# Attention without its division: the row sums' reciprocals kept in memory and applied to x where the feed-forward layer reads it

## The chip, the cores and the metric

The kernel runs on one core of one Trainium2 chip. The metric is the device time of one execution in microseconds (us), as the median of several runs. The core has a matrix engine (TensorE, PE), a vector engine (VectorE, DVE), a scalar engine (ScalarE, ACT), a general engine (GpSimd, POOL) and SyncE (SP), which here only issues DMA transfers. Each engine works through its own list of instructions in order; semaphores join the lists.

## The reference

```python
# attention: q, k, v are (4, 8, 576, 64); masked in blocks of 64
scores = scale * np.matmul(q, k.transpose(0, 1, 3, 2))
scores = np.where(mask, scores, -1000000000.0)
attn = np.exp(scores - np.max(scores, axis=-1, keepdims=True))
attn = attn / (np.sum(attn, axis=-1, keepdims=True) + 1e-09)
attn_out = np.matmul(attn, v)
x = attn_out.transpose(0, 2, 1, 3).reshape(2304, 512)
# feed-forward: w_in (512, 2048), w_out (2048, 512)
h = x @ w_in
g = np.where(h > 0.0, h, np.exp(np.minimum(h, 0.0)) - 1.0)
x = g @ w_out
# experts: one of 8 for each token where x @ w_skip > 0
out = x; out[do] = x[do] + gate * (relu(x[do] @ w1[e]) @ w2[e])
```

All of it is in float32.

## The kernel before

**Attention.** Two heads of a batch are a pair; there are 16 pairs, 4 for each of the 4 batches. One step of each engine's loop works on pair n and finishes the two pairs before it: TensorE makes the scores of n, turns the exponentials of n-1 and multiplies those of n-2 with v (`values`). ScalarE makes the exponentials with their row sums. VectorE makes the row maxima, the reciprocals of the row sums (`recips`), and copies turned tiles. The exponentials aren't divided. Instead the reciprocals, 9 columns of 128, are turned by TensorE and copied to `r_rows` (9 x 128, `recip_rows`), SyncE stores them to memory (`store_recips`, line 263) and loads them back repeated over the 64 partitions of each head into `r_sb` (`load_recips`, lines 271 and 274, four loads), and VectorE's `final` (line 443) multiplies the pair's sums in `o_ps` with `r_sb` into `attn_sb`, which SyncE stores to `attn_t` (line 257). `attn_t` is x turned: 512 rows (columns of x), 2304 tokens. There is one `o_ps`, one `r_sb` and one `attn_sb`, and TensorE may write the next `o_ps` only after `final` (`out_done`).

SyncE's step (`step` in `sync`) issues in this order: the part of w_in for this pair (line 279), q and k of pair n+3 (line 231, four loads), v of pair n (lines 250 and 252, three), the store of the reciprocals of n-1, the store of `attn_sb` of n-2, the four loads of reciprocals of n-1. GpSimd's step splits q and k of pair n+1 in a high and a low part (`qk_hi`, `qk_lo`, lines 343 and 346) and then the part of w_in (`wi_hi`, `wi_lo`, lines 354 and 359). TensorE's scores of a pair wait for its split.

**Feed-forward.** It runs over 6 blocks of 384 tokens. x of a block is loaded from `attn_t` in four row groups (`x_raw`, `load_x_rows`, line 35) and split in `xt_hi` (ScalarE, line 1537) and `xt_lo` (GpSimd, line 1137); for block 0 GpSimd does both within the attention's last steps (`x_parts`, lines 372 and 375). A block has 16 chunks f of the hidden layer. TensorE makes the hidden product of chunk f (`ff_hidden`, `h_ps`) and then the output product of chunk f-2 (`ff_output`, `out_ps`). ScalarE makes the exponential (`ex`, line 1520) and VectorE the rest and the low half `gt` (lines 1359, 1362, 1352). In block 0 w_out is loaded chunk by chunk (`load_wo`, line 1052, four buffers `w_raw`) and split by ScalarE (`wo_hi`, line 1585, two chunks ahead, ahead of that step's exponential in its list) and GpSimd (`wo_lo`). x of block b+1 is split at chunks 4, 6, 8 and 10 of block b (`X_AT`). The experts follow.

```python
        def final(n, i):
            wait(dve, pv_done, n + 1)
            wait(dve, r_in, R_LOADS * (n + 1))
            wait(dve, stored[1 - i], 16 * ((n + i) // 2))
            dve.tensor_tensor(attn_sb[:, :], o_ps[:, O0:O0 + S], r_sb[:, :], ALU.mult)\
               .then_inc(out_done, 1)
```

Of the kernel before, what the change touches and what calls it, by code (L numbers as in the profile page):

```python
# [21 lines left out]
P = 128  # L22
# [43 lines left out]

def attention_engines(nc, ctx, place, attn_t, wi, x_raw, x_in, xt0, x_hi_done, x_lo_done):

# [28 lines left out]
    WO, XT1, GT = LATER_AT  # L97
    R_LOADS = 64
    PIECES = [(j, max(j * P, a), b) for j in range(T) for a, b in ((0, O_SPLIT), (O_SPLIT, S)) if j * P < b]
# [4 lines left out]
    def sb(name, shape, dt):  # L104
        return place.enter_context(nc.sbuf_tensor(name, shape, dt))
# [33 lines left out]
    prob4 = sb("prob4", [P, S], F32)  # L139
    r_sb = sb("r_sb", [P, S], F32)  # L140
    vb.append(sb("v1", [P, T, 2, D], F32))
# [6 lines left out]
    half_row = sb("half_row", [P, P], BF16)  # L148

    r_dram = [nc.dram_tensor(f"recip_rows{i}", (COLS, P), F32, kind="Internal").ap() for i in range(2)]  # L150

# [23 lines left out]
    r_stored = sem("r_stored")  # L175
    r_in = sem("r_in")
    pv_done = sem("pv_done")
# [62 lines left out]
    def sync(sp, first_wo, next_wo):  # L240
# [19 lines left out]
        def store_recips(n, i):  # L260

            wait(sp, r_row_done, n + 1)
            sp.dma_start(r_dram[i], r_rows[:, :]).then_inc(r_stored, 16)

        def load_recips(n, i):

            wait(sp, out_done, n)
            wait(sp, r_stored, 16 * n + 16)
            for h in range(2):
                rows = HALVES[h]  # L270
                sp.dma_start(r_sb[rows, 0:FULL * P], r_dram[i][h * FULL:(h + 1) * FULL, :]  # L271
                             .rearrange("(o u) q -> o (u q)", o=1).broadcast_to([D, FULL * P]))\
                  .then_inc(r_in, 16)
                sp.dma_start(r_sb[rows, FULL * P:S], r_dram[i][COLS - 1:COLS, rows]  # L274
                             .broadcast_to([D, TAIL])).then_inc(r_in, 16)

# [5 lines left out]
        def step(kk, i):  # L282
            now, past, older, ahead = pair(kk, i), pair(kk, i, -1), pair(kk, i, -2), pair(kk, i, 3)
            first = isinstance(kk, int) and kk <= 0
            if now and not (first and now[0] == 0):
                load_wi(now[0])
            if ahead:
                load_qk(*ahead)
            if now and not first:
                load_v(*now)  # L290
            if past:
                store_recips(*past)
            if older:
# [25 lines left out]
        store(PAIRS - 2, 0)  # L319
        load_recips(PAIRS - 1, 1)  # L320
        next_wo()
        store(PAIRS - 1, 1)

    def gpsimd(pool):
# [60 lines left out]
    def vector(dve):  # L385
# [96 lines left out]

        all_pairs(step, -1, PAIRS + 1)(dve)
        return lambda: final(PAIRS - 1, 1)
# [84 lines left out]
    def tensor(pe, hidden):  # L569
# [138 lines left out]
        for m in range(PAIRS - 2, PAIRS):  # L708
# [12 lines left out]
    return dict(sync=sync, gpsimd=gpsimd, vector=vector, scalar=scalar, tensor=tensor, stored=stored,  # L721
                out_done=out_done, pv_done=pv_done, pairs=PAIRS, turned=tails_turned)

# [8 lines left out]
def experts(nc, x2_rows, table, meta, w1, w2, out, w1_raw, w1_in):  # L732
# [42 lines left out]
    with ExitStack() as ctx:  # L775
# [12 lines left out]

        x_hi_done, x_lo_done = sem("x_hi_done"), sem("x_lo_done")
        with ExitStack() as place:  # L790
# [5 lines left out]
            attend = attention_engines(nc, ctx, place, attn_t, wi, x_raw, xr_in, xt0, x_hi_done, x_lo_done)  # L796
# [4 lines left out]
        wo_raw = [spare[:, r // 2, r % 2] for r in range(WR)]  # L801
        ex = sb("ex", [P, 2, NB], F32)
        x2 = [sb(f"x2_{s}", [P, DM], F32) for s in range(TB)]
# [206 lines left out]
        def _(sp):  # L1010
            def load_x(b, ks=range(KC)):

                for k in ks:
                    wait(sp, x_lo_done, KC * (b - 1) + k + 1)
                    load_x_rows(sp, attn_t, k, b * NB, x_raw, xr_in)

            def store_x2(b):
# [46 lines left out]
            for stored in attend["stored"]:  # L1064
                sp.wait_ge(stored, 16 * attend["pairs"] // 2)
            load_x(1)
            load_gates()
            for f in range(2 * WR, FC):
# [157 lines left out]
        def _(dve):  # L1226
# [128 lines left out]
            def step(b, f):  # L1355
# [159 lines left out]
        def _(act):  # L1515
# [14 lines left out]
            def x_hi(b, k):  # L1530
                act.wait_ge(xr_in[k], 16 * (b + 1))
                if k == 0:
# [422 lines left out]
```

## Time and profile before

| | |
|---|---|
| median of 3 runs | 811.36 us (811.15 to 812.75) |
| the profiled execution | 812.12 us, span 810.3 us |
| busy, share of the span: PE, DVE, ACT, POOL | 94%, 63%, 43%, 30% |
| attention (to the last `r_rows` copy) | to 182.8 us |
| feed-forward, then experts | to about 617 us, then to the end |
| mean granted TensorE clock | 0.983 of full speed |
| DMA queue of SyncE (q1) | 96928 packets, 81.89 MB |

The profiled execution is 0.8 us above the median of the runs. The span is the time from the first to the last instruction of it. Times in the rows below are us from the start of the span. [...] A matmul counts as busy for longer when the clock is low, so a busy share doesn't tell a slow clock from work.

### The profile page before, as it was taken

The page shows a single profiled execution, that of the slowest core. Times are in us where ns is not written, and L with a number is a line of the kernel's source. Part 1 is how long each engine was busy: PE and PEld are TensorE (multiplying, and loading weights), DVE is VectorE, ACT ScalarE, POOL GpSimd, SP SyncE. Part 2 cuts the span into 40 slices and gives each one's busy share as a digit, 9 for nine tenths or more (in the row PEclk, how much of TensorE's full clock was granted, in tenths as well). Part 3 has the DMA queues.
Part 4 walks back from the last instruction along what each step waited for, and adds up shares of the span by engine and source line. Part 5 has one row for each costly group of instructions (what it writes and reads, how often), then busy time and mean ns, then how long its engine had stood idle before and what let it go on. Part 6 is the DMA issues. An engine that isn't in the chain of part 4 may idle for free.

```text
span 810.3 us, 15508 instructions
## 1 busy us (share of the span) xinstructions
PE 765.6 (94%) x5170; PEld 645.9 (80%) x5171; DVE 511.3 (63%) x1307; ACT 349.9 (43%) x830; POOL 245.3 (30%) x240
## 2 busy tenths in 40 slices
PE   5998888889999999999999999999997999999995
PEld 3777766668889888888988888898875777878884
DVE  3877677564333885687488488526755898377242
ACT  4877776663433222321322322223442776256241
POOL 4876676764440120120121012000112223213111
PEclk9999999799999999999999999999998999999999
DMA  9566666555252020210210200321333699164000
GB/s 159 141 166 168 161 166 181 134 154 150 77 179 79 20 72 1 89 30 1 78 30 11 79 1 27 121 88 53 112 131 105 225 334 352 46 225 149 26 21 9
DMA packets 102405, 88.16 MB, mean 109 GB/s; under 512 B 66164, under 2 KB 77828, under 8 KB 102224
## 3 DMA queue, kind: packets, MB, share of 16 engines
q1 hardware_dynamic: 96928, 81.89, 33.4%
q0 software_dynamic: 3056, 5.00, 1.8%
q10 hardware_dynamic: 2368, 0.59, 0.4%
q8 instruction: 30, 0.49, 0.2%
q14 instruction: 23, 0.19, 0.1%
HBM read 72.26 MB, written 18.34 MB: 112 GB/s over the span
## 4 chain that ended last, share of the span: by engine, by line
PE 77%; SPq 9%; DMA 4%; issue 4%; DVE 3%; ACT 1%; POOL 1%; DVEq 1%; POOLq 0%; ACTq 0%
PE h_ps L1695 12%; PE out_ps L1695 12%; PE h_ps L1696 11%; PE h_ps L1697 11%; PE out_ps L1697 11%; PE out_ps L1696 11%; SPq L231 3%; DMA recip_rows<-r_rows 3%; PE o_ps L672 2%; SPq L274 2%; SPq L271 1%; PE out_ps L1831 1%; SPq L250 1%; SPq L252 1%; PE o_ps L581 1%
## 5 line engine op out<-in xcount | busy, mean ns | idle before, releaser
L1520 ACT ACTIVATE ex<-h_ps 128x384 f32<-128x384 f32 x96 | 47.3, 493 | 272.4 <-PE h_ps L1697 272.4
L1695 PE MATMUL h_ps<-xt_hi,wi_hi 128*128 128x384 f32 x384 | 131.9, 343 | 0.2 <-POOL xt_lo L375 0.2
L1696 PE MATMUL h_ps<-xt_lo,wi_hi 128*128 128x384 f32 x384 | 129.7, 338 | 0.0
L1697 PE MATMUL h_ps<-xt_hi,wi_lo 128*128 128x384 f32 x384 | 129.7, 338 | 0.0
L1359 DVE TENSOR_SCALAR ex<-ex 128x384 f32<-128x384 f32 x96 | 37.0, 385 | 138.7 <-ACT ex L1520 137.5
L1695 PE MATMUL out_ps<-wo_hi,gt 128*128 128x512 f32 x288 | 114.5, 398 | 0.0
L1697 PE MATMUL out_ps<-wo_hi,gt 128*128 128x512 f32 x288 | 113.9, 395 | 0.0
L1696 PE MATMUL out_ps<-wo_lo,gt 128*128 128x512 f32 x288 | 113.3, 393 | 0.0
L529 ACT ACTIVATE prob<-s_ps,negmax 128x128 f32<-128x128 f32 (+2 forms) x144 | 77.8, 554 | 25.6 <-DVE negmax L391 23.9
L1241 DVE CUSTOM_DVE_ANT_0 x2t<-x,w_raw 128x512 bf16<-128x512 f32 x108 | 82.7, 806 | 0.4
L1137 POOL TENSOR_TENSOR xt_lo<-x_raw,xt_hi 128x384 fp32r<-128x384 f32 x20 | 28.3, 1416 | 156.2 <-ACT xt_hi L1537 156.1
L1695 PEld LDWEIGHTS h_ps<-xt_hi,wi_hi 128*128 128x128 f32 x384 | 72.2, 188 | 4.0 <-POOL xt_lo L375 0.5
L1696 PEld LDWEIGHTS h_ps<-xt_lo,wi_hi 128*128 128x128 f32 x384 | 72.2, 188 | 3.1
L1145 POOL DMA_INDIRECT route_table<-entry,slot x18 | 20.9, 1164 | 177.2 <-DVE slot L1320 161.0
L1697 PEld LDWEIGHTS h_ps<-xt_hi,wi_lo 128*128 128x128 f32 x384 | 72.1, 188 | 0.0
L1697 PEld LDWEIGHTS out_ps<-wo_hi,gt 128*128 128x128 f32 x288 | 54.1, 188 | 13.4
L1695 PEld LDWEIGHTS out_ps<-wo_hi,gt 128*128 128x128 f32 x288 | 54.1, 188 | 9.1 <-DVE gt L1352 0.8
L1696 PEld LDWEIGHTS out_ps<-wo_lo,gt 128*128 128x128 f32 x288 | 54.1, 188 | 8.9
L391 DVE TENSOR_REDUCE negmax<-s_ps 128x2 f32<-128x256 f32 (+1 forms) x64 | 50.8, 816 | 15.3 <-PE s_ps L659 15.2
L1362 DVE TENSOR_TENSOR ex<-h_ps,ex 128x384 f32<-128x384 f32 x96 | 53.5, 558 | 3.3
L1695 PE MATMUL out_ps<-wo_hi,ht_hi 128*128 128x512 f32 x120 | 50.3, 419 | 3.7 <-DVE ht_lo L1428 3.5
L1352 DVE TENSOR_TENSOR gt<-ex,gt 128x384 fp32r<-128x384 f32 x96 | 53.1, 554 | 0.0
(179 smaller groups left out, 1587.6 us busy)
## 6 DMA issues: line engine op xcount, KB each, us to landing
w_raw<-in_moe_w_dram SPq DMA_DIRECT2D x56, 512.0 KB, 4.8
raw_qk<-in_q_dram SPq DMA_DIRECT2D x32, 144.0 KB, 3.2
attn_t<-attn_sb SPq DMA_DIRECT2D x16, 288.0 KB, 2.2
x_raw<-attn_t SPq DMA_DIRECT2D x24, 192.0 KB, 2.4
out_dram<-x SPq DMA_DIRECT2D x18, 256.0 KB, 2.1
x_rows<-x SPq DMA_DIRECT2D x18, 256.0 KB, 2.4
v<-in_v_dram SPq DMA_DIRECT2D x32, 128.0 KB, 2.9
wi_raw<-in_moe_w_in_dram SPq DMA_DIRECT2D x16, 256.0 KB, 2.9
```

The costliest lines, as they stand in the source:

```text
L231: eng.dma_start(raw[i][rows, :, h, :], heads_of(t, n)[h].rearrange("(b p) d -> p b d", p=D))\
L391: dve.tensor_reduce(heads_cols(negmax, u), s_pair(u), AX_X, ALU.max, negate=True).then_inc(max_done, 1)
L529: act.activation(dst, src, ACT.Exp, bias=negmax[:, c:c + 1], accum_out=rowsum[i][:, c:c + 1]).then_inc(exp_done, 1)
L1137: pool.tensor_tensor(xtk(b % 2, 1, k), x_raw[k][:, :], xtk(b % 2, 0, k).bitcast(F32), ALU.subtract).then_inc(x_lo_done, 1)
L1241: ins = dve.tensor_tensor_reduce(dot_rows[:, ((E + 1) * t + e) % 2], x2[s][:, :], all_skip if e == E else all_gates[:, e, :], 1.0, 0.0, AL ...
L1352: dve.tensor_tensor(gt[:, f % 2, 1], ex[:, f % 2], gt[:, f % 2, 0].bitcast(F32), ALU.subtract).then_inc(g_lo_done, 1)
L1359: dve.tensor_scalar(e, e, 1.0, -1.0, ALU.min, ALU.add).then_inc(em_done, 1)
L1362: dve.tensor_tensor(e, h_ps[:, f % 2, 0:NB], e, ALU.max).then_inc(g_done, 1)
L1520: act.activation(ex[:, f % 2], h_ps[:, f % 2, 0:NB], ACT.Exp).then_inc(ex_done, 1)
L1695: pe.matmul(dst, stat[0], mov[0], start=start, stop=False, skip_group_check=True)
L1696: pe.matmul(dst, stat[0], mov[1], start=False, stop=False, skip_group_check=True)
L1697: return pe.matmul(dst, stat[1], mov[0], start=False, stop=stop, skip_group_check=True)
```

## The change

`final` becomes a copy: `attn_t` now holds undivided sums. The reciprocals of all pairs are kept in one array in memory, `recip_rows`, with a row of 9 x 128 for each pair. `load_recips` of the attention is gone with its four loads for each pair. Where x of a block has been loaded, SyncE loads the reciprocals of its tokens and of the two heads of that row group, repeated over 64 partitions for each head (`recip_row`, a new `load_recips`), and VectorE multiplies `x_raw` with them in place (`normalise`, 128 x 384, 24 times in all). ScalarE and GpSimd split x only after that (`x_norm`). A block's tokens lie in one, two or three pieces of `recip_rows`: block 0 and 3 need one load for each row group, block 2 and 5 two, block 1 and 4 three. Blocks 0 and 1 have a buffer for each row group (in `w1_raw`), the others one buffer for all four.

```diff
+def recip_row(r_rows, b, k):
+    PAIR_TOKENS, MAIN = 576, 512
+    for batch in range(4):
+        first = batch * PAIR_TOKENS
+        for a, z, at in ((0, MAIN, 0), (MAIN, PAIR_TOKENS, 2 * MAIN)):
+            lo, hi = max(first + a, b * X_TILES * P), min(first + z, (b + 1) * X_TILES * P)
+            if lo < hi:
+                row = r_rows[4 * batch + k:4 * batch + k + 1, at:at + 2 * (z - a)]
+                yield (slice(lo - b * X_TILES * P, hi - b * X_TILES * P),
+                       row.rearrange("o (h q) -> h o q", h=2)[:, :, lo - first - a:hi - first - a]
+                       .broadcast_to([2, P // 2, hi - lo]))
+def load_recips(sp, r_rows, b, k, dst, x_r_in):
+    for cols, src in recip_row(r_rows, b, k):
+        sp.dma_start(dst[:, cols], src).then_inc(x_r_in[min(b, 2)][k], 16)
+def normalise(dve, x, r, x_in, x_r_in, x_norm, b, k, loads):
+    dve.wait_ge(x_in[k], 16 * (b + 1))
+    dve.wait_ge(x_r_in[min(b, 2)][k], 16 * loads)
+    dve.tensor_tensor(x[k][:, :], x[k][:, :], r, ALU.mult).then_inc(x_norm, 1)
...
-            sp.dma_start(r_dram[i], r_rows[:, :]).then_inc(r_stored, 16)
-        def load_recips(n, i):
-            wait(sp, out_done, n)
-            wait(sp, r_stored, 16 * n + 16)
-            for h in range(2):
...
+            sp.dma_start(r_all[bass.ds(n, 1)].rearrange("o (c q) -> (o c) q", q=P), r_rows[:, :])\
+              .then_inc(r_stored, 16)
...
-            wait(dve, r_in, R_LOADS * (n + 1))
-            dve.tensor_tensor(attn_sb[:, :], o_ps[:, O0:O0 + S], r_sb[:, :], ALU.mult)\
-               .then_inc(out_done, 1)
+            dve.tensor_copy(attn_sb[:, :], o_ps[:, O0:O0 + S]).then_inc(out_done, 1)
...
-                pool.wait_ge(x_in[k], 16)
+                pool.wait_ge(x_norm, k + 1)
...
+            for k in range(KC):
+                load_r(1, k)
             load_gates()
...
+                for k in range(KC):
+                    if b and b < LAST and k < KC - 1:
+                        load_r(b + 1, k + 1)
+                    if b + 2 < BLOCKS:
+                        load_x(b + 2, [k])
                 if b + 2 < BLOCKS:
-                    load_x(b + 2)
+                    load_r(b + 2, 0)
...
+                if b < LAST and f + 1 in X_AT:
+                    k = X_AT.index(f + 1)
+                    normalise(dve, x_raw, x_r[b + 1][k], xr_in, x_r_in, x_norm, b + 1, k,
+                              recip_loads(r_all, b + 1, k))
...
-                act.wait_ge(xr_in[k], 16 * (b + 1))
+                act.wait_ge(x_norm, KC * b + k + 1)
```

SyncE's list at the head of pair 12 of the attention, before: the four loads of x of block 0, then the pair's own transfers. "128x384" is what one transfer writes, x3 that three follow each other, and "waits" names the semaphores.

```order
L35 DMA x_raw<-attn_t 128x384 [waits stored1,stored0]
L35 DMA x_raw<-attn_t 128x384 x3
L279 DMA wi_raw<-in_moe_w_in_dram 128x4x128 [waits wi_lo_done]
L231 DMA raw_qk<-in_q_dram 64x9x64 [waits tails_turned]
L231 DMA raw_qk<-in_q_dram 64x9x64
L231 DMA raw_qk<-in_k_dram 64x9x64 x2
L250 DMA v<-in_v_dram 128x4x64 [waits pv_done]
L250 DMA v<-in_v_dram 128x4x64
L252 DMA v<-in_v_dram 64x2x64
L263 DMA recip_rows<-r_rows 9x128 [waits r_row_done]
L257 DMA attn_t<-attn_sb 128x576 [waits out_done]
L271 DMA r_sb<-recip_rows 64x512 [waits r_stored,out_done]
```

The same place now. "w_raw<-recip_rows" are the new loads (the names of the buffers have lost their numbers, here it is `w1_raw`).

```order
L35 DMA x_raw<-attn_t 128x384 [waits stored1,stored0]
L35 DMA x_raw<-attn_t 128x384 x3
L85 DMA w_raw<-recip_rows 128x1x384 [waits r_stored]
L85 DMA w_raw<-recip_rows 128x1x384 x3
L300 DMA wi_raw<-in_moe_w_in_dram 128x4x128 [waits wi_lo_done]
L263 DMA raw_qk<-in_q_dram 64x9x64 [waits tails_turned]
L263 DMA raw_qk<-in_q_dram 64x9x64
L263 DMA raw_qk<-in_k_dram 64x9x64 x2
L282 DMA v<-in_v_dram 128x4x64 [waits pv_done]
L282 DMA v<-in_v_dram 128x4x64
L284 DMA v<-in_v_dram 64x2x64
L295 DMA recip_rows<-r_rows 9x128 [waits r_row_done]
```

Four new loads stand between the loads of x and the pair's own, and none follows the pair's stores.

SyncE's list after the attention now, from the last store of `attn_sb` to the loads of w_out's chunks from 8 on. Before, the loads of `gates` came right behind those of x.

```order
L289 DMA attn_t<-attn_sb 128x576 [waits out_done]
L35 DMA x_raw<-attn_t 128x384 [waits r_stored,x_lo_done,stored1,stored0]
L35 DMA x_raw<-attn_t 128x384 [waits x_lo_done] x3
L85 DMA w_raw<-recip_rows 128x1x128
L85 DMA w_raw<-recip_rows 128x1x64
L85 DMA w_raw<-recip_rows 128x1x192
...
L1075 DMA gates<-in_moe_w_gate_dram 128x4x8
L1076 DMA gates<-in_moe_w_skip_dram 128x4x1
L1092 DMA w_raw<-in_moe_w_out_dram 128x512 [waits wo_lo_done] x8
```

The three loads of the middle come four times, once for each row group: twelve transfers have been put ahead of w_out's.

## Rows read from the trace of the kernel before

**Rows 1.** The page's chain that ended last, by engine.

```profile
PE 77%; SPq 9%; DMA 4%; issue 4%; DVE 3%; ACT 1%; POOL 1%; DVEq 1%; POOLq 0%; ACTq 0%
```

**Rows 2.** Timeline of SyncE's queue, one pair: start, us, line, transfer.

```profile
94.21 0.39 SPq L279 DMA_DIRECT2D wi_raw<-in_moe_w_in_dram  x1
...
100.16 0.40 SPq L263 DMA_DIRECT2D recip_rows<-r_rows  x1
...
101.86 0.51 SPq L271 DMA_DIRECT2D r_sb<-recip_rows  x1
...
104.56 0.39 SPq L279 DMA_DIRECT2D wi_raw<-in_moe_w_in_dram  x1
```

**Rows 3.** Waits of the whole span: us in total, times, longest.

```profile
DVE attn_sb L443 <- DMA r_sb<-recip_rows: 18.0, 10, 3.1
```

**Rows 4.** Busy time by stretches: length, PE, PEld, DVE, ACT, POOL, PEclk, DMA.

```profile
23.95:51.07 27.12, 26.42 (x406) 20.48 (x404) 22.25 (x48) 23.52 (x78) 23.76 (x20) 1.00 0.63 151
...
94.71:104.45 9.74, 9.03 (x138) 7.00 (x135) 7.60 (x17) 7.70 (x26) 7.21 (x7) 1.00 0.64 165
...
136.44:148.25 11.81, 10.33 (x138) 8.44 (x136) 7.76 (x16) 7.80 (x27) 6.75 (x6) 0.86 0.94 196
148.25:162.29 14.04, 11.03 (x136) 8.89 (x134) 7.88 (x17) 7.76 (x26) 9.34 (x8) 0.76 0.41 121
```

**Rows 5.** Timeline of VectorE: copies of `r_rows`, one `final` between them.

```profile
51.07 0.28 DVE L427 COPY r_rows<-t_ps 9x128 f32<-9x128 f32 x1 [1.01 <-PE t_ps L581]
...
63.70 0.76 DVE L443 TENSOR_TENSOR attn_sb<-o_ps,r_sb 128x576 f32<-128x576 f32 x1 [2.04 <-DMA r_sb<-recip_rows]
...
136.44 0.28 DVE L427 COPY r_rows<-t_ps 9x128 f32<-9x128 f32 x1 [1.00 <-PE t_ps L581]
```

**Rows 6.** DMA in three stretches: 269 to 272, 182.9 to 185.2, 228.6 to 231.

```profile
DMA packets 144, 0.20 MB, mean 66 GB/s; under 512 B 16, under 2 KB 144, under 8 KB 144
...
q1 hardware_dynamic: 144, 0.20, 23.2%
...
x_raw<-attn_t SPq DMA_DIRECT2D x1, 192.0 KB, 2.2
...
DMA packets 72, 0.13 MB, mean 59 GB/s; under 512 B 9, under 2 KB 18, under 8 KB 71
...
DMA packets 160, 0.28 MB, mean 116 GB/s; under 512 B 24, under 2 KB 24, under 8 KB 160
```

**Rows 7.** The table by stretches again, a large load: last columns DMA share, GB/s.

```profile
232.40:238.00 5.60, 5.60 (x29) 4.96 (x28) 1.99 (x5) 2.33 (x5) 1.67 (x2) 1.00 0.91 342
```

**Rows 8.** Timeline of GpSimd: w_in's part, then the split of the next pair.

```profile
142.59 1.04 POOL L354 TENSOR_TENSOR wi_hi<-wi_raw,one 128x512 f32 x1 [4.73 <-DMA wi_raw<-in_moe_w_in_dram]
...
145.11 1.04 POOL L343 TENSOR_TENSOR qk_hi<-qk_f,one 128x512 fp32r<-128x512 f32 x1
...
148.90 1.67 POOL L346 TENSOR_TENSOR qk_lo<-qk_f,qk_hi 128x704 fp32r<-128x704 f32 x1
```

**Rows 9.** Timeline of VectorE in block 1 of the feed-forward.

```profile
283.69 0.36 DVE L1359 TENSOR_SCALAR ex<-ex 128x384 f32<-128x384 f32 x1 [0.27 <-ACT ex L1520]
...
284.56 0.55 DVE L1352 TENSOR_TENSOR gt<-ex,gt 128x384 fp32r<-128x384 f32 x1
```

**Rows 10.** Timelines at the attention's end: VectorE, GpSimd, TensorE.

```profile
174.56 1.00 DVE L435 COPY pt<-t_ps 128x384 f32<-128x384 f32 x2
...
174.54 0.83 POOL L372 TENSOR_TENSOR xt_hi<-x_raw,one 128x384 fp32r<-128x384 f32 x1
...
178.37 0.44 PE L1695 MATMUL h_ps<-xt_hi,wi_hi 128*128 128x384 f32 x1 [0.22 <-POOL xt_lo L375]
```

**Rows 11.** Timelines behind the attention: TensorE's last values, ScalarE's list.

```profile
184.96 2.93 PE L672 MATMUL o_ps<-pt,v 128*64 128x256 f32 x28
...
203.61 0.62 ACT L1585 ACTIVATE wo_hi<-w_raw 128x512 fp32r<-128x512 f32 x1
...
207.00 0.49 ACT L1520 ACTIVATE ex<-h_ps 128x384 f32<-128x384 f32 x1 [2.76 <-PE h_ps L1697]
```

More of the change, by code:

```diff
@@ L64, in attention, with recip_loads, attention_engines @@
     given.update(q=q, k=k, v=v, w_in=w_in)
-def attention_engines(nc, ctx, place, attn_t, wi, x_raw, x_in, xt0, x_hi_done, x_lo_done):
+def recip_row(r_rows, b, k):
[12 more added lines that the diff above has]
+        sp.dma_start(dst[:, cols], src).then_inc(x_r_in[min(b, 2)][k], 16)
+def recip_loads(r_rows, b, k):
+    return sum(1 for b1 in range(min(b, 2), b + 1) for _ in recip_row(r_rows, b1, k))
+def normalise(dve, x, r, x_in, x_r_in, x_norm, b, k, loads):
+    dve.wait_ge(x_in[k], 16 * (b + 1))
+    dve.wait_ge(x_r_in[min(b, 2)][k], 16 * loads)
+    dve.tensor_tensor(x[k][:, :], x[k][:, :], r, ALU.mult).then_inc(x_norm, 1)
+def attention_engines(nc, ctx, place, attn_t, wi, x_raw, x_in, xt0, x_hi_done, x_lo_done, r_all, x_r, x_r_in,
+                      x_norm):
     q, k, v, w_in = (given[n] for n in ("q", "k", "v", "w_in"))
@@ L139, in attention_engines @@
     prob4 = sb("prob4", [P, S], F32)
-    r_sb = sb("r_sb", [P, S], F32)
+    sb("pad_r", [P, S], F32)
     vb.append(sb("v1", [P, T, 2, D], F32))
@@ L148, in attention_engines @@
     half_row = sb("half_row", [P, P], BF16)
-    r_dram = [nc.dram_tensor(f"recip_rows{i}", (COLS, P), F32, kind="Internal").ap() for i in range(2)]
     s_ps = place.enter_context(nc.psum_tensor("s_ps", [P, 4 * BANK], F32))
@@ L312, in sync @@
             load_x_rows(sp, attn_t, c, 0, x_raw, x_in)
+        sp.wait_ge(r_stored, 16 * GROUP)
+        for c in range(len(x_raw)):
+            load_recips(sp, r_all, 0, c, x_r[0][c], x_r_in)
         for m in range(PAIRS - 4, PAIRS):
@@ L481, in step @@
                 turned_halves(*now, 2, t_ps, t2_done, t2_out)
-        all_pairs(step, -1, PAIRS + 1)(dve)
+        all_pairs(step, -1, PAIRS - 1)(dve)
+        for m in range(2):
+            for c in range(m * len(x_raw) // 2, (m + 1) * len(x_raw) // 2):
+                normalise(dve, x_raw, x_r[0][c], x_in, x_r_in, x_norm, 0, c, recip_loads(r_all, 0, c))
+            step(PAIRS // 2 - 1 + m, 1 - m)
         return lambda: final(PAIRS - 1, 1)
@@ L721, in attention_engines @@
     return dict(sync=sync, gpsimd=gpsimd, vector=vector, scalar=scalar, tensor=tensor, stored=stored,
-                out_done=out_done, pv_done=pv_done, pairs=PAIRS, turned=tails_turned)
+                out_done=out_done, pv_done=pv_done, pairs=PAIRS, turned=tails_turned,
+                r_stored=r_stored, s_done=(s_done, SCORES * PAIRS))
 def feed_forward(nc, attn_t, wi, x_raw, x_in, w_out, w_skip, w_gate, out, x2_rows, table, meta,
@@ L789, in experts @@
         x_hi_done, x_lo_done = sem("x_hi_done"), sem("x_lo_done")
+        r_all = nc.dram_tensor("recip_rows", (N // (TB * P) * 8 // 3, 9 * P), F32, kind="Internal").ap()
+        x_r_in, x_norm = [[sem(f"x_r_in{b}_{k}") for k in range(KC)] for b in range(3)], sem("x_norm")
+        x_r_cols = w1_raw[:, :, :, :].rearrange("p j o f -> p (j o f)")
+        x_r = [[x_r_cols[:, (b * KC + k) * NB:(b * KC + k + 1) * NB] for k in range(KC)] for b in range(2)]
         with ExitStack() as place:
@@ L795, in experts @@
             assert nc.sbuf_base == given["base"]
-            attend = attention_engines(nc, ctx, place, attn_t, wi, x_raw, xr_in, xt0, x_hi_done, x_lo_done)
+            attend = attention_engines(nc, ctx, place, attn_t, wi, x_raw, xr_in, xt0, x_hi_done, x_lo_done,
+                                       r_all, x_r, x_r_in, x_norm)
         assert nc.sbuf_base == given["base"]
@@ L801, in experts @@
         wo_raw = [spare[:, r // 2, r % 2] for r in range(WR)]
+        x_r += [[spare[:, 2, 1, 0:NB]] * KC for b in range(2, BLOCKS)]
         ex = sb("ex", [P, 2, NB], F32)
@@ L1015, in load_x, with load_r @@
                     load_x_rows(sp, attn_t, k, b * NB, x_raw, xr_in)
+            def load_r(b, k):
+                if b > 1 and (b, k) > (2, 0):
+                    sp.wait_ge(x_norm, KC * b + k)
+                load_recips(sp, r_all, b, k, x_r[b][k], x_r_in)
             def store_x2(b):
@@ L1065, in _ @@
                 sp.wait_ge(stored, 16 * attend["pairs"] // 2)
+            sp.wait_ge(attend["r_stored"], 16 * attend["pairs"])
             load_x(1)
+            for k in range(KC):
+                load_r(1, k)
             load_gates()
```

12 lines of the change are left out of this document (1 added, 11 removed).

## The prediction

> **What bounds the kernel now.** Start with the page's chain of waits: 77% of the span is TensorE, 9% is SyncE's queue (SPq) and 4% DMA [rows 1]. The feed-forward blocks and the experts are TensorE's, so the queue's share must lie in the attention. The timeline of SyncE there shows why. In one pair (a step of the loop) it issues 14 transfers of about 0.6 us, and between the store of the reciprocals at 100.16 and their first load back at 101.86 it waits for the store to land; from one load of w_in to the next are 10.35 us [rows 2]. The table of waits names the receiver: VectorE waits 18.0 us in 10 places for r_sb [rows 3], and TensorE, which needs `o_ps` back, with it. The table by stretches, cut at the copies of `r_rows` (one for each pair), gives the price. Three pairs at the start take 27.12 us, 9.04 each, with TensorE at full clock; a pair of the loop takes 9.74 with TensorE busy 9.03; two later ones take 11.81 and 14.04, with the granted clock at 0.86 and 0.76 and TensorE "busy" 10.33 and 11.03 for the same 136 to 138 matmuls [rows 4]. [...] TensorE's own need is 9.05 to 9.2 us a pair; I take 9.15.
>
> **What it removes.** Four loads (2.5 us of SyncE's queue) and the wait for the store's round trip, for each pair. SyncE is left with 10 transfers, under 7.65 us (from w_in's load at 94.21 to 101.86, where its first load back stood [rows 2]). That is under 9.15, so TensorE becomes the pace. From the copy at 51.07 to the one at 136.44 lie eight pairs [rows 5], 85.4 us; 8 x 9.15 = 73.2. That is **-12.2 us**. Were only VectorE's waits given back and the clock not, it would be 10.4 (seven of the ten waits lie there, of 0.67 to 2.04 us; one of the longest stands in [rows 5]); were each pair as fast as 9.04, 13.1. The next two pairs (25.85 us, to 162.29) would give 7.55 more, if nothing new came there. Making the product a copy (576 wide) changes nothing: VectorE has idle time around it.
>
> **What it adds: loads of another form.** The new loads come from `recip_row`. Their source has the dimensions 2 x 64 x n (head, repeated 64 times, columns), into 128 partitions. Every load of the kernel before begins with 64 or 128 rows on both sides. No row of before has a load that begins with 2, so its cost must be bounded. What rows do show is how a transfer is spread. A load of x_raw leaves 144 packets: 128 of data and 16 under 512 B, one end mark for each of 16 DMA engines. In the stretch with the store of 9 rows there are 9 packets under 512 B, and in the one with a 128-row load beside the 8-row store of the gates, 24 = 16 + 8 [rows 6]. So the number of engines follows the outer rows, it isn't always 16. A load whose outer dimension is 2 then has two engines, 64 packets each.
> Price of one load of 192 KB (1536 B in 128 partitions): spread over 16, a landing of 2.2 us like x_raw's [rows 6] and next to no queue. On two engines: x_raw's 144 packets took 23.2% of 16 engines in 3.0 us [rows 6], 11.1 engine-us, so 5.6 us on each of two; by the best stream of the trace (342 GB/s at a share of 0.91, 23.5 GB/s an engine [rows 7]) 4.2 us. I take 4.8, between them, since queued packets have no starts between them. What I choose is the two-engine form: the end marks speak for it.
> [...]
>
> **First jam, in the attention.** [...] At the head of pair 12 SyncE issues four loads of x and now four of reciprocals: 4 x 4.8 = 19.2 us on two rings. Set t = 0 at the first of these. Their data starts behind x at 1.5, ends at 20.7. The load of w_in's part 12, issued at 2.5, lands at 21.6 instead of 5.4. Behind it GpSimd is stopped, in order: `wi_hi` and `wi_lo`, then the split of pair 14, 2.5 and 5.5 us [rows 8], so the split is ready at 29.6. TensorE would begin pair 14 at 17.5 (two pairs of 9.15, less 0.8 that SyncE is behind pair 12's start). It waits 12.1 us; with the `r_rows` and `attn_sb` stores, which VectorE waits for in pair 13, also behind the jam but due sooner (about 9 us late), I keep 12.4. The two pairs take 18.3 + 12.4 = 30.7 instead of 25.85: **+4.9 us**.
>
> **The end of the attention.** VectorE now multiplies x by the reciprocals, 0.55 us each by the equal subtraction [rows 9], and GpSimd's `x_parts` wait for it. The first two products fit before pair 15's first maximum or delay it by 0.5 us, which ScalarE absorbs. The last two come after the copies of `pt` that end at 175.56. GpSimd's `xt_hi` started at 174.54 and now can at 176.15; TensorE was already waiting for the last `xt_lo` (0.22 us) [rows 10]. **+1.6 us**.
>
> **Second jam, in block 0.** The last pair's values end at 187.9 [rows 11] (times of before from here). VectorE's copy is done at 188.7 rather than 191.1, the store lands about 192.0, x of block 1 is issued to 193.8. Then come 12 loads for four rows (512, 256 and 768 B in 128 partitions), the same bytes: with the small pieces 5.0 us a row, 20.0 us from 194.3. The load of `wo` 8 stands behind them and lands at 215.8. ScalarE is in order: `wo_hi` 8 (203.61) stands ahead of the exponential of chunk 6 (207.00) [rows 11]. So these two, VectorE's two steps and the difference for chunk 5 end at 215.8 + 2.6 = 218.4. TensorE wants chunk 5's half at 211.0, 4.2 us after chunk 6's hidden product. **+7.4 us**. In blocks 1 to 4 the loads go one row at a time: 5.0 + 1.2 + 1.5 = 7.7 us after the product before it, and the next is due two chunks (8.4 us) later; VectorE has 0.27 us or more idle in its fullest chunks [rows 9] and some 2 us before TensorE notices. Nothing.
> Each jam leaves TensorE idle for long, and the slowed clock behind waits cost 1.3 us (10.33 against 9.03 busy [rows 4]): **+2.6 us**.
>
> **Sum.** -12.2 + 4.9 + 1.6 + 7.4 + 2.6 = +4.3 on the profiled execution's 812.1: 816.4. The median of the runs lies 0.8 below it, so 815.6. With 4.2 us a load and no clock loss it is 808, with 5.6 it is 822; 808 to 823 is the forecast's own range.
>
> **The rivals.**
> 1. **The new loads spread over 16 engines** (the other side: faster). Then no jam: ten pairs from 51.07 to 162.29, 111.2 us, become 91.5, -19.7, and +1.6 remains: 812.1 - 18.1 - 0.8 = 793.2 (790.5 to 799). For it: the destination does begin with 128. Against: the end marks. It decides as soon as one load's landing is under 3 us.
> 2. **Only the first jam reaches TensorE**, because `wo` 8 gets past or comes earlier: 815.6 - 7.4 - 1.3 = 806.9. Against it stands ScalarE's order.
> 3. **Pace.** SyncE gone, something else keeps the pairs at 10.67 (85.4 / 8), say the store of `attn_sb`. The pairs with no wait at 9.04 speak against it. With jams 827.8.
>
> **How the numbers follow.** Forecast 0.60, first rival 0.27, second 0.10, third 0.03. About 0.2% (1.6 us) can be told from no change, so slower is above 813.0 and faster below 809.7. Of the forecast's 0.60, 0.48 lie above, 0.08 between, 0.04 below. Slower 0.48 + 0.03 = 0.51; faster 0.04 + 0.27 + 0.09 = 0.40; same 0.09. The range must take in most of the first rival: 792 to 823.
>
> **What would show it.** Right: pairs of 9.1 to 9.2 us up to pair 11 and a clock of 1.00 there; end marks of two for each new load; landings of 5 us and, in the queue, up to 20; GpSimd waiting 15 us or more for `wi_raw` once, then TensorE idle some 12 us; ScalarE waiting some 12 us for `wo` 8 in block 0. Wrong: landings of 2.5 us for the new loads (then 793), a jam that ends before its data is due, products in blocks 1 to 4 that wait for their reciprocals, or pairs above 9.5 us.

## The result, and the profile after

The changed kernel takes 817.52 us (median of 4 runs, 816.81 to 818.23), the kernel before beside it 811.72 us (4 runs): 1.007 times as long, with an interval of 1.0053 to 1.0087. So it is slower by 5.8 us, more than the 0.2% that can be told from nothing; the forecast was 815.6. In the later runs the kernel before spread from 807.1 to 817.2 us (45 runs, with medians of 811.8, 813.4 and 812.8 in three groups), so its single executions reach as high as the changed kernel's, and its medians do not. Each experiment below is compared with the kernel before beside it. The profiled execution took 817.13 us with a span of 815.1 us, against 812.1 and 810.3.

The chain of waits of the page after has moved as the pace of the pairs did: SyncE's queue is down from 9% to 6% and DMA from 4% to 2% [rows 1]. A new line stands in it, L85, the loads of the reciprocals.

```profile
PE 80%; SPq 6%; ACT 4%; DVE 3%; issue 3%; DMA 2%; DVEq 1%; POOL 1%; POOLq 0%; ACTq 0%
```

The table by stretches, cut at the copies of `r_rows` again: eight pairs, the two pairs of the first jam one by one, pair 14, and the end of the attention. The columns are the stretch, its length, the busy time of each engine with its instructions, the granted clock of TensorE as a share of its full speed (PEclk), the DMA share and GB/s.

```profile
51.15:123.89 72.74, 71.31 (x1075) 55.90 (x1073) 60.21 (x128) 60.60 (x201) 60.78 (x49) 1.00 0.64 165
123.89:144.78 20.89, 9.55 (x142) 7.25 (x138) 7.52 (x17) 7.83 (x27) 5.24 (x5) 0.83 0.39 106
144.78:155.85 11.07, 10.65 (x128) 8.94 (x130) 7.81 (x17) 7.54 (x24) 10.59 (x9) 0.70 0.33 94
155.85:164.78 8.93, 8.22 (x118) 6.26 (x118) 7.92 (x16) 6.80 (x23) 6.91 (x8) 1.00 0.34 98
164.78:178.21 13.43, 10.37 (x123) 7.51 (x122) 6.35 (x13) 7.54 (x19) 8.11 (x8) 1.00 0.42 124
```

Eight pairs take 72.74 us, 9.09 each, with TensorE at full clock; before they took 85.4 [rows 5]. Then one pair takes 20.89, in which TensorE works 9.55, and the next 11.07 at a clock of 0.70: 31.96 for what took 25.85 before [rows 4]. The end takes 13.43, before 11.55.

Who waits in the 20.89, by the timelines of GpSimd, TensorE and VectorE (start, duration, engine, line, operation, and in brackets the idle time ahead with what ended it):

```profile
140.65 1.04 POOL L375 TENSOR_TENSOR wi_hi<-wi_raw,one 128x512 f32 x1 [15.33 <-DMA wi_raw<-in_moe_w_in_dram]
```
```profile
145.20 1.08 PE L604 MATMUL t_ps<-ident,prob 64*128 64x64 f32 x15 [11.56 <-DVE r_rows L448]
```
```profile
144.78 0.28 DVE L448 COPY r_rows<-t_ps 9x128 f32<-9x128 f32 x1 [12.82 <-DMA recip_rows<-r_rows]
```

GpSimd stands 15.3 us for the part of w_in, as forecast. TensorE, though, stands 11.6 us for VectorE's copy of `r_rows`, and VectorE 12.8 us for the store of the `r_rows` before it. The prediction had named the split on GpSimd as the last wait and this store as "due sooner". SyncE's queue shows what it had not counted:

```profile
118.12 1.81 SPq L35 DMA_DIRECT2D x_raw<-attn_t  x4
119.97 7.79 SPq L85 DMA_DIRECT2D w_raw<-recip_rows  x4
127.81 3.35 SPq L300 DMA_DIRECT2D wi_raw<-in_moe_w_in_dram  x1
131.20 4.75 SPq L263 DMA_DIRECT2D raw_qk<-in_q_dram  x2
136.00 3.42 SPq L263 DMA_DIRECT2D raw_qk<-in_k_dram  x2
...
141.54 0.51 SPq L295 DMA_DIRECT2D recip_rows<-r_rows  x1
```

An issue itself is held up. Four loads of reciprocals take 7.79 us of the issuing engine, one load of w_in 3.35 and four of Q and K 8.2, where one took 0.4 to 0.8 in a pair of the kernel before (0.39 to 0.51 for those in [rows 2]). So the store, ready when VectorE had copied at 123.89, was only issued at 141.54.

Behind the attention the second jam stands where it was expected:

```profile
188.66 16.59 SPq L85 DMA_DIRECT2D w_raw<-recip_rows  x12
...
207.23 10.40 SPq L1092 DMA_DIRECT2D w_raw<-in_moe_w_out_dram  x5
```
```profile
211.04 0.63 ACT L1637 ACTIVATE wo_hi<-w_raw 128x512 fp32r<-128x512 f32 x1 [11.20 <-DMA w_raw<-in_moe_w_out_dram]
```
```profile
213.65 0.77 PE L1747 MATMUL out_ps<-wo_hi,gt 128*128 128x512 f32 x1 [6.01 <-DVE gt L1400]
```

Twelve loads hold SyncE for 16.6 us, the load of `wo` 8 is issued behind them, ScalarE waits 11.2 us for it, and TensorE 6.0 us for the half of the difference behind that. All of block 0 by the table, from the last copy of `r_rows` to the first exponential of block 1, first before and then after, and behind them 6.35 us of the changed kernel right behind that wait:

```profile
182.78:249.45 66.67, 66.67 (x351) 59.52 (x352) 26.40 (x53) 22.45 (x49) 26.32 (x30) 1.00 0.39 123
```
```profile
178.21:254.89 76.68, 69.88 (x351) 61.69 (x352) 30.58 (x57) 22.27 (x48) 26.58 (x30) 0.96 0.36 116
...
213.65:220.00 6.35, 6.35 (x18) 5.48 (x19) 3.54 (x4) 1.37 (x3) 3.62 (x3) 0.53 0.27 83
```

TensorE has 351 matmuls in both. Before it is busy without a gap; now it stands 6.8 us, and is "busy" 3.2 us longer for the same work, since right behind the wait it was granted a clock of 0.53. So the second jam costs 10.0 us. The blocks after it lose nothing: from the first exponential of block 1 to the last one of block 5 it is 338.34 us before and after.

A simple bookkeeping for all kernels here: each span is cut at the first copy of `r_rows` (22.5 to 24 us from the start), at the last one, at the first exponential of block 1, and at its end. The numbers are the starts of these instructions in the timelines of VectorE and ScalarE of each profiled execution.

| kernel | first to last copy, us | last copy to block 1 (block 0), us | block 1 to the end, us | span, us |
|---|---|---|---|---|
| before | 158.8 | 66.7 | 560.9 | 810.3 |
| after | 154.2 | 76.7 | 560.2 | 815.1 |
| every new load as two halves | 142.7 | 72.2 | 561.1 | 798.4 |
| block 0's new loads as halves | 141.9 | 75.6 | 559.3 | 799.4 |
| block 1's new loads as halves | 155.0 | 72.1 | 561.3 | 811.1 |
| every one as halves, block 1's asked for early | 142.7 | 66.7 | 560.2 | 793.4 |
| the same, products ahead of pair 14 | 141.0 | 66.7 | 561.1 | 791.4 |

The change won 4.6 us in the attention and lost 10.0 in block 0. In every kernel 338.3 to 338.4 us of the fourth column are blocks 1 to 5. The rest, the experts in the main, takes 220.9 to 223.0 us, and no edit touches it: three more executions of the kernel before with loads added (experiments 1, 8 and 9) have 220.5, 222.4 and 220.5 where this one has 222.5. So some 2 us of a span are the spread of the experts, and some 1.5 more lie ahead of the first copy. Each row is one execution: with unchanged code in the attention and block 0 (experiment 1) the kernel before has 157.9 and 66.9 us in the second and third column, so differences there tell from about 1 us in the attention and from some tenths in block 0.

### The profile page after: what moved, and what is told of

Read it like the earlier page. It is cut to its first block, busy times and chain, and to the rows that moved or that the text cites. A ratio compares the mean times of both kernels' runs of the same rounds, so it can differ in the third digit from the quotient of the medians.

```text
span 815.1 us, 15528 instructions
## 1 busy us (share of the span) xinstructions
PE 765.1 (94%) x5170; PEld 644.9 (79%) x5171; DVE 523.1 (64%) x1331; ACT 348.0 (43%) x830; POOL 244.9 (30%) x240
## 4 chain that ended last, share of the span: by engine, by line
PE 80%; SPq 6%; ACT 4%; DVE 3%; issue 3%; DMA 2%; DVEq 1%; POOL 1%; POOLq 0%; ACTq 0%
PE out_ps L1747 11%; PE h_ps L1747 11%; PE h_ps L1748 11%; PE h_ps L1749 11%; PE out_ps L1748 11%; PE out_ps L1749 11%; PE o_ps L695 5%; SPq L85 3%; PE s_ps L679 2%; ACT prob L552 2%; PE t_ps L604 2%; PE out_ps L1883 1%; PE s_ps L674 1%; SPq L263 1%; ACT pt L536 1%
## 5 line engine op out<-in xcount | busy, mean ns | idle before, releaser
L552 ACT ACTIVATE prob<-s_ps,negmax 128x128 f32<-128x128 f32 (+2 forms) x144 | 77.8, 556 | 11.6 <-DVE negmax L412 10.2
L1747 PEld LDWEIGHTS out_ps<-wo_hi,gt 128*128 128x128 f32 x288 | 54.5, 189 | 16.6 <-issue 7.4
L1400 DVE TENSOR_TENSOR gt<-ex,gt 128x384 fp32r<-128x384 f32 x96 | 55.0, 572 | 0.0
```

The costliest lines, as they stand in the source:

```text
L552: act.activation(dst, src, ACT.Exp, bias=negmax[:, c:c + 1], accum_out=rowsum[i][:, c:c + 1]).then_inc(exp_done, 1)
L1400: dve.tensor_tensor(gt[:, f % 2, 1], ex[:, f % 2], gt[:, f % 2, 0].bitcast(F32), ALU.subtract).then_inc(g_lo_done, 1)
L1747: pe.matmul(dst, stat[0], mov[0], start=start, stop=False, skip_group_check=True)
```

## The experiments

**1. What one load costs.** The kernel before with six loads of 192 KB in block 2, where the queue is quiet; they differ only in the outermost dimension of the source, and each is waited for.

```diff
+                if b == 2:
+                    for i, outer in enumerate((128, 2, 4, 8, 16, 128)):
+                        src = attn_t[0:outer, 0:NB]
+                        if outer < P:
+                            src = src.unsqueeze(1).broadcast_to([outer, P // outer, NB])
+                        sp.dma_start(spare[:, 2, 1, 0:NB], src).then_inc(probed, 16)
+                        sp.wait_ge(probed, 16 * (i + 1))
```

Expected: 

> The kernel before, with six loads of 192 KB added in SyncE's idle time in block 2 of the feed-forward, one after the other, each waited for: source outer dimension 128, 2, 4, 8, 16 and 128 rows, each repeated to fill 128 partitions of an unused buffer. Theory (two engines): the number of DMA engines is the outer dimension, up to 16. With 11.1 engine-us a load, data takes 5.6, 2.8, 1.4 and 0.7 us on 2, 4, 8, 16 engines, and a landing is that plus 1.5: about 7, 4.3, 2.9, 2.2, and 2.2 for 128. End marks (packets under 512 B) 2, 4, 8, 16 and 16. Rival (spread over 16 whatever the source): all six land in 2.2 to 2.5 us with 16 marks. The time of the whole stays within 1 us of before by either.

The view of DMA, for the stretch of one load each: the packets with their kinds, and the queue's share of 16 engines. First outermost 2 (32 packets of another queue are in that stretch), then 4, 8 and 128:

```profile
DMA packets 162, 0.20 MB, mean 38 GB/s; under 512 B 34, under 2 KB 162, under 8 KB 162
...
q1 hardware_dynamic: 130, 0.20, 11.4%
```
```profile
DMA packets 132, 0.20 MB, mean 61 GB/s; under 512 B 4, under 2 KB 132, under 8 KB 132
...
q1 hardware_dynamic: 132, 0.20, 18.0%
```
```profile
DMA packets 136, 0.20 MB, mean 103 GB/s; under 512 B 8, under 2 KB 136, under 8 KB 136
...
q1 hardware_dynamic: 136, 0.20, 30.2%
```
```profile
DMA packets 144, 0.20 MB, mean 89 GB/s; under 512 B 16, under 2 KB 144, under 8 KB 144
...
q1 hardware_dynamic: 144, 0.20, 34.2%
```

Beside 128 packets of data stand 2, 4, 8 and 16 of under 512 B on this queue. Read as the prediction reads them, they are an end mark for each engine that took part. No view names the engines, but the busy share in 40 slices of each stretch speaks for it: it is 1 tenth of the 16 in most slices with 2 marks, 2 tenths with 4, and 4 to 6 tenths with 8. The time by that count: 11.4% of 16 engines over 5.25 us are 9.6 engine-us, 4.8 on each of two. With 4 it is 2.3 us (18.0% of 16 over 3.2 us, by 4), with 8 it is 1.15 (30.2% of 16 over 1.9 us, by 8), and with 16 it is 0.6 (25.5% of 16 over 2.4 us, by 16, from 379.2 us on, with 144 packets and 16 marks). So the 4.8 us that the prediction chose between 4.2 and 5.6 holds. The changed kernel's own load shows the same where it stands almost alone, in block 3: between 338.5 and 345 us there are one load of x (144 packets, 16 end marks) and one of reciprocals.

```profile
DMA packets 276, 0.42 MB, mean 64 GB/s; under 512 B 18, under 2 KB 274, under 8 KB 274
...
q1 hardware_dynamic: 274, 0.39, 19.9%
```

274 less 144 are 130, and 18 less 16 are 2: two engines, and the first rival falls. The one run of the probe took 810.41 us, within the spread of the kernel before (807.1 to 815.4 us beside it). With 128 rows at the destination in every load, it was the source's outermost dimension that decided: 2, 4, 8 and 16 marks with as many rows, and 16 with 128. What an outermost dimension that is no power of two does in such a load was not tried.

**2 to 4. The same loads, spread.** Each new load is written as two of 64 rows, one for each half of the partitions; bytes, product and waits stay. Once for all blocks (`HALVED` is 0 to 5), once for block 0 alone (the first jam), once for block 1 alone (the second).

```diff
     for cols, src in recip_row(r_rows, b, k):
-        sp.dma_start(dst[:, cols], src).then_inc(x_r_in[min(b, 2)][k], 16)
+        if b in HALVED:
+            for h in range(2):
+                sp.dma_start(dst[h * 64:(h + 1) * 64, cols], src[h]).then_inc(x_r_in[min(b, 2)][k], 16)
+        else:
+            sp.dma_start(dst[:, cols], src).then_inc(x_r_in[min(b, 2)][k], 16)
```

Expected for all blocks: 

> The changed kernel, with each new load of reciprocals written as two, one for each head, 64 x n into 64 partitions (the form of the old loads of r_sb): 96 loads instead of 48, the same bytes. Theory (two engines jam the queue): both jams go; the pairs take 9.1 us to the end; the 24 issues of 0.6 us ahead of w_out's chunk 8 cost up to 3 us in block 0. 793 to 799 us. Rival (the loss comes from the number of transfers put ahead of the others in SyncE's list, not from their form): twice the transfers, so the loss grows: 820 us or more. Rival (the multiplication on VectorE costs it): unchanged, 817.

For block 0: 

> The changed kernel with the two-load form only for the reciprocals of block 0, at the head of pair 12 in the attention. Theory (two engines): only the first jam goes. From the r_rows copy of pair 11 to that of pair 13 the changed kernel took 31.96 us and should take 18.3: 13.7 us less, 803 to 805. GpSimd's wait of 15.3 us for wi_raw and VectorE's of 12.8 for the store of r_rows go. Rival (number of transfers): four more at that place, 818 or more. If VectorE's or GpSimd's wait was not what stopped TensorE, it stays above 810.

For block 1: 

> The changed kernel with the two-load form only for the reciprocals of block 1, behind the attention. Theory (two engines): only the second jam goes, in which TensorE stood 6.8 us for gt (0.8 and 6.0) and lost about 0.5 to 1.3 us by its clock. The 24 issues (14.4 us) leave chunk 8 of w_out late by some 4 us at ScalarE, of which 2 to 3 reach TensorE. So 3 to 7 us less: 810 to 814. Rival (number of transfers): 12 more ahead of w_out, 822 or more.

Measured: all blocks 800.57 us, 0.9856 of before (0.9826 to 0.9886); block 0 alone 802.08, 0.9882 (0.9845 to 0.992); block 1 alone 813.84, 1.0024 (1.0006 to 1.0043). All blocks is 1.4% under the kernel before, and 2.1% under the changed kernel (0.9856 / 1.007). So the form of the loads, not their bytes, number or product, made the change slow: the rivals' 818 and more, and 817, are out. Two of the three lie outside what was expected: 800.6 is above 793 to 799, where up to 3 us were counted for the 24 issues and block 0 lost 5.5 (below), and 802.1 is under 803 to 805. With halves the two pairs of the first jam take 18.9 us (copies at 122.29, 131.81 and 141.20) instead of 31.96, 13 us for the first jam alone. By the table, the run for block 0 gained 12.3 us in the attention and 1.1 in block 0; another 1.0 is the experts' spread. The run for block 1 gained 4.6 us in block 0 and kept the first jam (31.1 us, copies at 122.54 and 153.61).

The second jam did not go with the form of its loads. In the kernel with halves everywhere SyncE issues 24 loads, and ScalarE still waits:

```profile
175.23 15.66 SPq L90 DMA_DIRECT2D w_raw<-recip_rows  x24
```
```profile
ACT wo_hi L1644 <- DMA w_raw<-in_moe_w_out_dram: 11.3, 2, 8.8
...
PE out_ps L1754 <- DVE gt L1407: 4.0, 1, 4.0
```
```profile
165.15:237.31 72.16, 68.19 (x351) 60.44 (x352) 29.23 (x57) 22.14 (x47) 25.77 (x29) 0.98 0.40 123
```

15.7 us of issuing against 16.6 before: twice as many loads, each at 0.65 us, near the 0.54 us that is the median of the changed kernel's 48. ScalarE's longest wait for `wo` 8 fell only from 11.2 to 8.8 us. Of the jam's 10.0 us in block 0, 5.5 are left (72.16 for 66.67): 4.0 of waiting and 1.5 of slowed clock.

**5. Block 1's loads asked for early.** They need only batches 0 and 1 and a buffer that is free, so they can go out in the attention's last four pairs, six halves behind each. (The wait for the stores at the head of pair 12 now asks for those of both batches.)

```diff
         for m in range(PAIRS - 4, PAIRS):
             step(m // 2, m % 2)
+            load_recips(sp, r_all, 1, m - PAIRS + 4, x_r[1][m - PAIRS + 4], x_r_in)
...
             load_x(1)
-            for k in range(KC):
-                load_r(1, k)
```

Expected: 

> The kernel with each new load as two loads of 64 rows, and block 1's reciprocals (24 of these loads) asked for in the attention's last four pairs, six behind each, where SyncE has 3 to 5 us free in each pair, instead of ahead of the load of wo 8. Theory (what is left of the second jam is SyncE's issue: 24 loads took 15.7 us and ScalarE waited 8.8 us for wo 8, TensorE 4.0 us for VectorE's half of the difference): both waits go, and about 1.3 us of slowed clock with them: 800.6 - 4.0 - 1.3 = 795.3 us, between 794 and 797.5. Rival (24 more issues in pairs 12 to 15 hold up the loads of V, w_in and the stores there): the waits move into the attention, 799 to 803.

Measured 794.72 us (793.62 to 795.98), 0.9762 of before (0.9738 to 0.9787; the kernel before took 813.41 beside it), inside the theory's bounds. Block 0 fell from 72.2 to 66.7 us, what it took before the change, and the attention stayed at 142.7. SyncE's spare time in the attention, which the change had made, carries the 24 issues at no cost there. The table by stretches has the end of the attention, and then block 0 with TensorE without a gap:

```profile
151.38:166.47 15.09, 12.02 (x123) 8.43 (x122) 6.36 (x14) 7.28 (x17) 11.12 (x11) 0.89 0.46 137
...
166.47:233.16 66.69, 66.69 (x351) 59.55 (x352) 27.97 (x57) 22.16 (x48) 24.78 (x29) 1.00 0.41 122
```

The first of these rows shows what is left: the end of the attention takes 15.09 us, at a clock of 0.89, where the kernel before took 11.55.

**6. The products earlier.** All four products of block 0 stand ahead of pair 14's step in VectorE's order.

```diff
-            for c in range(m * len(x_raw) // 2, (m + 1) * len(x_raw) // 2):
+            for c in range(len(x_raw) if m == 0 else 0):
                 normalise(dve, x_raw, x_r[0][c], x_in, x_r_in, x_norm, 0, c, recip_loads(r_all, 0, c))
```

Expected: 

> The kernel before this one (halves, block 1's reciprocals early), and all four of VectorE's products for block 0 ahead of pair 14's step, where two of them stood ahead of pair 15's. Theory (the end of attention costs what GpSimd's last xt_hi waits for these products, 1.9 us in the kernel with halves): the last stretch between the r_rows copies falls from 15.0 to about 13 us, the time by 1.8, to about 793.5, between 792 and 796. Rival (the two products delay pair 14's first maximum by 1.1 us, and TensorE waits there instead): no gain, within 1 us of the kernel without it.

```profile
140.74:152.25 11.51, 8.25 (x116) 6.21 (x114) 11.51 (x18) 5.70 (x20) 11.02 (x10) 1.00 0.49 137
152.25:163.66 11.41, 9.97 (x123) 7.82 (x124) 5.51 (x13) 8.08 (x22) 7.62 (x9) 1.00 0.49 150
```

The end fell to 11.41 us at full clock, but the pair before it rose from 9.53 to 11.51, with VectorE busy all through: 24.62 us for the two became 22.92. So both theories have a part: of the 3.7 us won at the end 2.0 came back on VectorE. The runs give 794.92 us (0.9766, 0.9741 to 0.9791), no gain over the kernel without it. In the profiled executions 1.7 us are won up to the last copy, block 0 is the same (66.69), and 0.8 is lost in the experts, which is their spread. Whether the 1.7 us are real is not shown: the five runs of each kernel spread over more than 2 us.

**7. Two buffers for the stores.** The changed kernel with two `r_rows` and two `attn_sb` in turn, so that the store's late landing holds nobody.

```diff
-            wait(dve, r_stored, 16 * n)
-            dve.tensor_copy(r_rows[:, :].rearrange("c (s w) -> c s w", s=2), ...)
+            wait(dve, r_stored[i], 16 * ((n - i) // 2))
+            dve.tensor_copy(r_rows[i].rearrange("c (s w) -> c s w", s=2), ...)
```

Expected: 

> The changed kernel as it stands (loads that begin with 2), but with two buffers in turn for r_rows and two for attn_sb, so that VectorE's copies wait for the store of two pairs before. Theory A (in the first jam both chains are late: the store of r_rows, behind which TensorE stands from 133.6 to 144.8 us, and the load of w_in with GpSimd's split of pair 14 behind it, which ends at 148.6, when TensorE needs it at 150.1): the first wait falls away, TensorE comes to the scores of pair 14 at 138.7 and waits there for the split until 148.6 instead; gain 1.4 us, 816.1, between 815 and 817.5. Theory B (the store is the jam's whole cost): the stretch of two pairs falls from 32 to about 21 us and the time to 807, between 805 and 810.

Measured 816.85 us (10 runs), 1.0045 of before (1.0024 to 1.0066; the kernel before took 813.41 beside it). Theory B's 805 to 810 is out. The time lies in theory A's bounds, but the two pairs did not gain its 1.4 us. The wait for the store is gone (`r_rows` is copied at 125.08 and 134.22, at the full pace), and TensorE waits for two others instead:

```profile
144.71 1.12 PE L606 MATMUL o_ps<-ident,raw_qk 64*128 64x64 f32 x16 [7.48 <-DMA raw_qk<-in_k_dram]
150.09 0.80 PE L676 MATMUL s_ps<-qk_f 64*128 64x128 f32 x4 [4.26 <-POOL qk_lo L369]
```

7.5 us for the load of K of the next pair, which theory A had not named, then 4.3 for GpSimd's split. The next copy comes at 157.01: the two pairs (125.08 to 157.01) take 31.93 us, with one buffer 31.96. Behind one jam stood three chains that end within a few microseconds of each other, and taking away the last one showed the next.

**8 and 9. The jam alone.** The kernel before, with four loads of 192 KB behind the loads of x at the head of pair 12, into a free buffer, waited for by nobody in the attention; `ROWS` is 2 in one and 16 in the other.

```diff
+        for c in range(len(x_raw)):
+            sp.dma_start(spot[:, c * 384:(c + 1) * 384],
+                         attn_t[0:ROWS, 0:384].unsqueeze(1).broadcast_to([ROWS, P // ROWS, 384]))\
+              .then_inc(given["spot_in"], 16)
```

Expected with 2: 

> The kernel before, with four loads of 192 KB more, whose source is 2 rows x 64 times x 384 columns, behind the loads of x at the head of pair 12, into a buffer that nothing uses until later; nothing waits for them in the attention. Theory (two DMA engines hold 19 us of packets, and everything that SyncE issues behind them waits): the store of r_rows is issued about 23 us after the head, the split of pair 14 is ready about 30 us after it, and the stretch of two pairs grows from 25.9 to some 37 us: +11.5, 823 us, between 820 and 827. Rival (loads that nobody waits for cost only their issue and their bytes): +1 to +3.

Expected with 16: 

> The same four loads of 192 KB in the kernel before, with a source of 16 rows x 8 times x 384 columns. Theory (16 rows outermost go over all 16 engines, 0.7 us a load in the probe): within 0.2% of the kernel before, 811 to 813.5. Rival (the repeated rows or the bytes are what costs): as much as with 2 rows.

Measured: 829.21 us with 2, 1.0192 of before (1.0144 to 1.024), and 815.59 with 16, 1.0035 (1.0014 to 1.0057). SyncE's queue in both, first with 2:

```profile
138.34 8.37 SPq L316 DMA_DIRECT2D w_raw<-attn_t  x4
146.75 3.79 SPq L280 DMA_DIRECT2D wi_raw<-in_moe_w_in_dram  x1
...
160.51 0.51 SPq L264 DMA_DIRECT2D recip_rows<-r_rows  x1
```
```profile
139.55 2.53 SPq L316 DMA_DIRECT2D w_raw<-attn_t  x4
142.13 0.59 SPq L280 DMA_DIRECT2D wi_raw<-in_moe_w_in_dram  x1
...
148.54 0.51 SPq L264 DMA_DIRECT2D recip_rows<-r_rows  x1
```

Same bytes, same destination, same place, nobody waiting for the data: the store of `r_rows` is issued 22.2 us behind the first of these loads with 2 rows, and 9.0 us with 16. The longest landing of a load of w_in is 12.4 us with 2 rows and 5.0 with 16 (4.3 in the kernel before, with a median of 2.9). The two pairs take 39.1 us (copies at 138.08 and 177.17) and 28.1 (138.28 and 166.33), where they took 25.85. Both runs lie above what was expected, 829 for 820 to 827 and 815.6 for at most 813.5. Of the first, the profiled execution has a span 14.3 us above that of before: 13.2 are in these two pairs and 1.5 in the eight ahead of them, where nothing was added (86.85 for 85.37; with 16 rows they took 86.53). It was also the fastest of the four, 2.5 us under their median. The second says that even well spread loads cost 2 to 3 us at the head of pair 12 of this kernel, 2.2 in these two pairs; I put that down to the four issues, 2.5 us of SyncE where it was still the bound. Nor is it the repeating that costs: each half of experiments 2 to 6 reads one row 64 times, and in experiment 2 the two pairs took 18.9 us.

## Why the prediction was right

Direction, size and place came out, 815.6 against 817.5. By its steps:

- **What goes.** Eight pairs at 9.15 us were forecast, 73.2; they took 72.74. The reading of [rows 2 to 4], that SyncE's round trip cost itself and then clock, was right: TensorE is busy 71.31 of 72.74 us at a clock of 1.00. Before, it was busy 74.69 of 85.37, at 0.96: of the 12.6 us won 9.2 are waits and 3.4 are clock.
- **Two engines for a load.** Right: the changed kernel's load has two end marks, and experiment 1 has the 4.8 us, for a load alone in the queue. The reason given for 4.8, that queued packets have no starts between them, is shown by no run.
- **First jam.** 30.7 us and 1.3 of clock were forecast for the two pairs, 31.96 came: TensorE stood 11.8 us, where a wait of 12.4 was counted, and was busy 20.20, where two of the eight pairs ahead take 17.83, so the clock (0.83 and 0.70) cost 2.4. That a load issued behind the jam waits for it, and so lands at 21.6 (and `wo` 8 at 215.8), was the author's estimate, which no row of before shows. In the run w_in's part 12 landed 12.6 us after its issue, against a median of 2.8, and GpSimd took it up at 140.65, 22.5 us after the first load of x at 118.12. The size was right, the last link not: the prediction let TensorE wait for GpSimd's split; in the run it waited for VectorE, which waited for the store. It counted what a late *transfer* holds up and took SyncE's issues at 0.6 us behind the jam, while the issues themselves stood too. That the number came out all the same is luck in part, since the chains lie close together: experiment 7 shows that without the store's wait the load of K and the split make the two pairs just as long.
- **End of the attention.** +1.6 forecast, 13.43 for 11.55 us measured, +1.9. GpSimd's `xt_hi` waited 2.55 us for VectorE's product there.
- **Second jam.** Forecast +7.4 of waiting and 1.3 of clock, 8.7; measured 6.8 and 3.2, 10.0. The waiting was read rightly: the prediction had `wo` 8 land at 215.8 in the times of before; the attention ends 4.6 us earlier now, so 211.2, and ScalarE took it up at 211.04. The clock was the term taken too small, 1.3 from one pair of [rows 4]; TensorE's busy time for the same 351 matmuls grew by 3.2. The cause was described too simply here too: halves took away the two engines but only 1 us of the 16.6 us of issuing (the loads of w_out's chunks landed within 4.9 us once they were issued), and won 4.5 of the 10.0 us (experiment 2); the other 5.5 went when the issues did (experiment 5).
- **Products in blocks 1 to 4.** Nothing forecast, nothing seen: 338.34 us with and without them.
- **The sum.** Forecast +4.3 in the profiled execution, measured +4.8. Attention -12.2 + 4.9 + 1.6 + 1.3 = -4.4, measured -4.6; block 0 +8.7, measured +10.0; the experts' spread took 0.6 back. That it came so close is luck in part: the clock behind the two jams cost 5.6 us where 2.6 were counted, and the waits (18.6 for 19.8) and the pairs (-12.6 for -12.2) made up for some of it.

The first rival (spread over 16, 793.2 us) was false of the change as written. Its price was near what spread loads give once they are out of w_out's way: 794.7 in experiment 5, with the attention's end at 15.09 us. It had counted no time for SyncE's issues ahead of `wo` 8; halves make 24 of them, and then it is 800.6. The second rival (only the first jam) is refuted by ScalarE's 11.2 us for `wo` 8 and the third (pace stays at 10.67) by the 9.09 us a pair.

## What to carry to other kernels

Look at the outermost dimension of a broadcast source before anything else: 192 KB took 4.8 us with two rows outermost and 1.15 with eight (experiment 1, as busy time of each engine), and four such transfers with two rows that nobody waited for still held up what was issued behind them on that queue, by some 13 us more than with 16 (experiments 8 and 9: 22.2 and 9.0 us to the issue of the store). When a change frees the issuing engine in one stage, spend the slack on the issues of the next stage: that, with halved loads, turned +0.7% into -2.4%. And when several chains stand behind one jam, price the jam by its length, not by the chain that ends last; removing one of them left the two pairs at 31.93 us. Behind each long wait count the slowed clock too: here it cost 2.4 us (at 0.83 and 0.70 in the two pairs) and 3.2 (0.96 over block 0, 0.53 right behind the wait), by TensorE's busy time for equal work.

## What the runs showed of the hardware

- An issue on SyncE's queue is not always 0.5 to 0.6 us. The fourth of four loads with two rows outermost, at 123.2 us, took 4.6 us to issue:

```profile
L85 SPq DMA_DIRECT2D w_raw<-recip_rows x48: 504/537/4603, 120.0 to 490.4; - x48
```

  The median of 48 is 0.54 us. The issues of other loads behind them were slow too (w_in's took 3.35 us, one of Q 2.79, where the changed kernel's medians are 0.40 and 0.64), and so was what stood behind in SyncE's order: the store with 9 rows was issued at 141.54, 17.65 us after the copy that it stores.
- A load with the outermost dimension 2, alone in the queue, takes about the same engine time as one with 4 or 8 (9.6, 9.2 and 9.2 engine-us for 192 KB in experiment 1): what differs is over how many engines it is spread, by 2, 4 and 8 end marks. The load of 128 different rows took more, 12.0 (34.2% of 16 over 2.2 us).
- The granted clock of the same 123 matmuls differed. In the kernel of experiment 5 the end of the attention ran at 0.89 behind 3 us of gaps, in that of experiment 6, with gaps of 1.4 us, at 1.00; they took 12.02 and 9.97 us. In the changed kernel the same stretch, also with 3 us of gaps, ran at 1.00 (10.37 us busy). What decides between these is open.
